# Two dense layers by Strassen's scheme: seven products of half blocks in place of eight, layer one ahead of layer two, squares held in DRAM

## The reference

```
h = x @ w_in          # 3072x512 by 512x2048
g = relu(h) ** 2
out = g @ w_out       # 3072x2048 by 2048x512
```

## Time and profile before

| what | value |
|---|---|
| median of three runs | 915.57 us |
| span of the profiled execution | 919.5 us |
| the profiled execution's own device time | not recorded beside its span |
| dense stage in it | 391.03 to 915.49 us |
| TensorE busy | 902.2 us, 98% |
| DVE, ACT busy | 473.0 and 423.6 us |
| DMA moved | 99.55 MB |

### The profile page before, as it was taken

How to read it: one execution, slowest core, us unless ns; L and a number is a source line. 1 busy time by engine, 2 the same in 40 slices (tenths; PEclk the granted TensorE clock), 3 DMA queues, 4 the chain that set the end, 5 groups by cost and what they waited for, 6 DMA issues and landing times.

```text
span 919.5 us, 17240 instructions
## 1 busy us (share of the span) xinstructions
PE 902.2 (98%) x5248; PEld 734.5 (80%) x5249; DVE 473.0 (51%) x1431; ACT 423.6 (46%) x978; POOL 92.2 (10%) x146
## 2 busy tenths in 40 slices
PE   9999999989899999999999999999999999999998
PEld 7878777767688887888888888888888888888886
DVE  5787899876566678763242224222422332243224
ACT  7888999855566668552232113211322221232123
POOL 3112222224222223100000000000000000000000
PEclk9999999999999999999999999999999999999999
DMA  5556775185677669740012003100400040004001
GB/s 200 172 166 201 234 230 172 69 302 199 222 251 248 224 220 357 260 96 0 1 52 41 1 0 75 17 0 0 91 0 0 0 91 0 0 0 91 0 0 46
DMA packets 87463, 99.55 MB, mean 108 GB/s; under 512 B 56189, under 2 KB 56317, under 8 KB 87408
## 3 DMA queue, kind: packets, MB, share of 16 engines
q1 hardware_dynamic: 81120, 83.07, 29.0%
q0 software_dynamic: 6000, 15.49, 4.9%
q10 hardware_dynamic: 288, 0.34, 0.1%
HBM read 77.72 MB, written 25.56 MB: 112 GB/s over the span
## 4 chain that ended last, share of the span: by engine, by line
PE 89%; issue 3%; DMA 3%; ACT 2%; DVE 2%; ACTq 1%; POOLq 1%; POOL 0%; DVEq 0%; SPq 0%
PE bank L1220 29%; PE bank L1193 28%; PE bank L1102 6%; PE bank L1083 6%; PE bank L930 4%; PE bank L985 4%; PE bank L958 4%; PE bank L996 1%; DMA routed<-pad_row 1%; PE bank L1091 1%; ACT prob L703 1%; PE bank L1010 1%; PE bank L978 1%; PE bank L1075 1%; DMA x_raw<-routed 1%
## 5 line engine op out<-in xcount | busy, mean ns | idle before, releaser
L1591 DVE TENSOR_TENSOR g<-relu_c 128x512 f32<-128x512 f32 x96 | 66.5, 693 | 340.1 <-ACT relu_c L873 340.1
L873 ACT ACTIVATE relu_c<-bank 128x512 f32<-128x512 f32 x96 | 57.5, 599 | 371.1 <-PE bank L1193 371.1
L1220 PE MATMUL bank<-w_hi,g_lo 128*128 128x512 f32 x384 | 150.1, 391 | 0.0
L1193 PE MATMUL bank<-x_hi,w_lo 128*128 128x512 f32 x384 | 149.6, 390 | 0.0
L1220 PE MATMUL bank<-w_hi,g_hi 128*128 128x512 f32 x384 | 149.4, 389 | 0.0
L1220 PE MATMUL bank<-w_lo,g_hi 128*128 128x512 f32 x384 | 149.4, 389 | 0.0
L1193 PE MATMUL bank<-x_hi,w_hi 128*128 128x512 f32 x384 | 149.4, 389 | 0.0
L1193 PE MATMUL bank<-x_lo,w_hi 128*128 128x512 f32 x384 | 146.5, 389 | 0.0
L703 ACT ACTIVATE prob<-score,neg_max 128x264 f32<-128x264 f32 (+1 forms) x192 | 94.0, 496 | 14.2 <-DVE neg_max L1283 14.1
L1546 DVE TENSOR_TENSOR w_lo<-w_raw,w_hi x70 | 82.0, 1221 | 10.5 <-ACT w_hi L816 7.1
L1220 PEld LDWEIGHTS bank<-w_hi,g_lo 128*128 128x128 f32 x384 | 72.1, 188 | 17.2 <-DVE g_lo L1598 2.5
(11 more groups left out here) (151 smaller groups left out, 1304.3 us busy)
## 6 DMA issues: line engine op xcount, KB each, us to landing
w_raw<-in_weights SPq DMA_DIRECT2D x80, 512.0 KB, 5.8
q_in<-in_qT SPq DMA_DIRECT2D x24, 256.0 KB, 3.3
v_in<-in_v SPq DMA_DIRECT2D x24, 256.0 KB, 3.6
x_rows<-x_row SPq DMA_DIRECT2D x24, 256.0 KB, 3.2
x_row<-x_rows SPq DMA_DIRECT2D x96, 64.0 KB, 2.5
k_in<-in_kT SPq DMA_DIRECT2D x23, 264.0 KB, 3.6
x_res<-routed POOLq DMA_DIRECT2D x15, 260.0 KB, 6.4
x_raw<-routed POOLq DMA_DIRECT2D x14, 260.0 KB, 6.2
```

The source lines that it names most:

```text
L873: eng.activation(relu_c[:, f % 2, :], hc_ps[f % 2][:, :], ACT.Relu).then_inc(s_crelu, 1)
L1193: return eng.matmul(hc_ps[f % 2][:, :], w[f // UNIT][:, f % UNIT, wcols], x[:, c, :], start=begins, stop=ends)
L1220: ins = eng.matmul(yc_ps[s][:, :], gg[:, f % 2, s * P:(s + 1) * P], w[f // UNIT][:, f % UNIT, DM:CH], start=(f == 0 and n == 0), stop=(f = ...
L1591: eng.tensor_tensor(g[:, f % 2, :], relu_c[:, f % 2, :], relu_c[:, f % 2, :], ALU.mult).then_inc(s_cg, 1)
```

## The change

`x` and `w_in` are cut into 2x2 blocks: token halves of 512, halves of the inner dimension of 256, column halves. With A the weights and B the tokens' blocks, sums of blocks are formed ahead, seven products are taken in place of eight, and the results are put together from them (Winograd's form). The same is done for the squares and `w_out`.

Layer one runs in 12 steps `t` (3 groups of 1024 tokens by 4 quarters of the hidden dimension). A step has seven products of 12 matmuls. Products 1 and 2 go to the banks `pa`, 5 and 3 to `pc`, 6 and 7 to `pb`, 4 to `pd`; the second one of a pair adds to what the first has left, after DVE or ACT has read it. Per step `p1_copy` (ACT) brings product 1 to `q1`; DVE makes `u2`, `u3_z22`, `z21`, `z12` in `q1` to `q3`; ACT makes ReLU and square of blocks 11, 22, 21 and 12 in place; and SP stores the four (128x1024 f32, 512 KB each) to `g_rows` in DRAM. `q1` and `q2` may be written again when their store has landed (`s_st21`, `s_st12`).

Layer two runs afterwards in 3 groups of 7 products of 4 units of 12 matmuls. SP loads the squares back (`chain_g`, `b12_g`, `stream_g`), DVE forms the block sums `t1` to `t4` and, per unit, the lower part (`unit_lower`); ACT makes the upper part (`unit_upper`), with a ring of three. Outputs are turned by DVE and stored in pieces of 128 bytes (`store_y`, four DMAs of 64 KB for each of 24 halves).

Of the weights, the first half of `w_in` is loaded during the last experts in place of the former units, and DVE makes its four sums (`first_sums`, ahead of the last expert). The other six slices pass through `w_in8`: SP loads one (`load_slice`, two DMAs of 512 KB), GpSimd makes four sums of 128x512 (`weight_sums`), ACT and DVE split seven blocks in three pieces (`slice_upper`, `slice_lower`) at t = 1, 2, 9, 10, 11 and after the last step. Slices for layer two overwrite those of layer one.

The core of the diff (block layout, buffers and layer two are left out):

```diff
+PRODUCTS = (1, 5, 6, 2, 7, 4, 3)
+LATER = {p: n + 1 for n, p in enumerate(PRODUCTS)}
+OPENING = (1, 2, 5, 6, 7, 4, 3)
+STEPS, QUARTERS, PIECES = 12, 4, ((1, 3), (3, 5), (5, 8))
...
+        PAIR = {"a": (0, 1), "c": (4, 5), "b": (6, 7), "d": (2, 3)}
+        pa, pc, pb, pd = (banks[:, n:m + 1, :] for n, m in PAIR.values())
+        BANK_OF = {1: "a", 2: "a", 5: "c", 3: "c", 6: "b", 7: "b", 4: "d"}
...
+            def store_g(t, blk, q, made, done):
+                eng.wait_ge(made, 2 * t + 2)
+                eng.dma_start(g_rows[t // QUARTERS, blk, t % QUARTERS, :, :], q[:, :, :].rearrange("p j t -> p (j t)")).then_inc(done, 16)
...
+            load_slice(0)
             eng.wait_ge(s_bscatter, tiles * 16 + 16)
             close(eng)
             eng.wait_ge(s_cturn, 4)
+            for c in range(DC):
+                load_x(0, 1, c, first_in[c], s_cx[c])
...
+            x_order = ((0, 0), (0, 1), (1, 0), (1, 1), (0, 2), (0, 3), (1, 2), (1, 3))
+            for t in range(STEPS):
+                if t in (2, 5):
+                    if t == 2:
+                        eng.wait_ge(s_wpl, 6)
+                    else:
+                        eng.wait_ge(s_xl, x_made(1, 3))
+                    for n, (token_half, c) in enumerate(x_order):
+                        load_x((t + 2) // 3, token_half, c, x_in[n], s_xin[n // 2])
+                if t == 9:
+                    eng.wait_ge(s_xl, x_made(2, 3))
+                    load_slice(2)
+                if t in (10, 11):
+                    load_slice(t - 7)
+                if t == STEPS - 1:
+                    for n in range(4):
+                        eng.wait_ge((s_st11, s_st12, s_st21, s_st22)[n], 16 * QUARTERS)
+                    load_chain(0, 0)
+                    load_chain(0, 1)
+                store_g(t, B11, q4, s_g11, s_st11)
+                if t == 1:
+                    eng.wait_ge(s_wpl, 3)
+                    load_slice(1)
+                if t in (9, 10):
+                    eng.wait_ge(s_wpl, 3 * (t - 6))
+                if t == STEPS - 1:
+                    load_chain(0, 2)
+                    load_chain(0, 3)
+                    eng.wait_ge(s_wpl, 15)
+                    load_slice(5)
+                store_g(t, B22, q3, s_g22, s_st22)
+                if t == STEPS - 1:
+                    load_b12(0, 0)
+                    load_b12(0, 1)
+                store_g(t, B21, q1, s_g21, s_st21)
+                if t == STEPS - 1:
+                    load_b12(0, 2)
+                    load_b12(0, 3)
+                store_g(t, B12, q2, s_g12, s_st12)
...
+            def weight_sums(k):
+                eng.wait_ge(s_win, 32 * k + 32)
+                a21, a11, s1, s2, a12, s3, a22, s4 = (w_in8[:, n, :] for n in range(8))
+                eng.tensor_tensor(s1, a21, a22, ALU.add).then_inc(s_wsum, 1)
+                eng.tensor_tensor(s3, a11, a21, ALU.subtract).then_inc(s_wsum, 1)
+                eng.wait_ge(s_wsum, 4 * k + 1)
+                eng.tensor_tensor(s2, s1, a11, ALU.subtract).then_inc(s_wsum, 1)
+                eng.wait_ge(s_wsum, 4 * k + 3)
+                eng.tensor_tensor(s4, a12, s2, ALU.subtract).then_inc(s_wsum, 1)
+            for k in range(6):
+                weight_sums(k)
...
+            def slice_upper(k, piece):
+                first, end = PIECES[piece]
+                s = (k + 2) % 4
+                if k >= 2:
+                    eng.wait_ge(s_one, halves(s + 8, 3 if k < 5 else (5, 2, 3)[piece]))
+                eng.wait_ge(s_wsum, 4 * k + 4)
+                eng.activation(w_hi[s // 2][:, first:end, s % 2 * SUPER:s % 2 * SUPER + SUPER], w_in8[:, first:end, :], ACT.Copy).then_inc(s_wph, 1)
+            def p1_copy(t):
+                eng.wait_ge(s_one, halves(t, 1))
+                wait(eng, s_st21, 16 * t)
+                eng.activation(q1[:, :, :], pa, ACT.Copy).then_inc(s_p1, 1)
...
+            eng.wait_ge(s_bscatter, tiles * 16 + 16)
+            close(eng)
+            for t in range(STEPS):
+                p1_copy(t)
+                if t == 0:
+                    block11(0)
+                    for p in (5, 6, 7, 4, 3):
+                        x_upper(0, p, x_source(0, p))
+                if t in (3, 7):
+                    x_upper((t + 1) // 4, 1, x_source(1, 1))
+                    x_upper((t + 1) // 4, 5, x_source(1, 5))
+                if t in (4, 8):
+                    x_upper(t // 4, 4, x_source(1, 4))
+                    x_upper(t // 4, 3, x_source(1, 3))
+                if t in (1, 2, 9, 10, 11):
+                    for piece in range(3):
+                        slice_upper({1: 0, 2: 1, 9: 2, 10: 3, 11: 4}[t], piece)
+                if t == STEPS - 1:
+                    unit_upper(0, 1, 0)
+                if t > 0:
+                    block11(t)
+                if t in (3, 7):
+                    x_upper((t + 1) // 4, 6, x_source(1, 6))
+                if t == STEPS - 1:
+                    unit_upper(0, 1, 1)
+                block22(t)
+                if t in (3, 7):
+                    x_upper((t + 1) // 4, 2, x_source(1, 2))
+                block21(t)
+                if t in (3, 7):
+                    x_upper((t + 1) // 4, 7, x_source(1, 7))
+                if t == STEPS - 1:
+                    unit_upper(0, 1, 2)
+                    slice_upper(5, 0)
+                block12(t)
+            slice_upper(5, 1)
+            slice_upper(5, 2)
...
+                if t >= 1:
+                    if p == 1:
+                        eng.wait_ge(s_g11, 2 * t - 1)
+                    elif p == 5:
+                        eng.wait_ge(s_z12, t)
+                    elif p == 6:
+                        eng.wait_ge(s_u3, 2 * t)
+                    elif p == 4:
+                        eng.wait_ge(s_z21, t)
+                if p == 2:
+                    eng.wait_ge(s_p1, t + 1)
+                elif p == 7:
+                    eng.wait_ge(s_u2, t + 1)
+                for j in range(2):
+                    if p == 3:
+                        eng.wait_ge(s_z22, 2 * t + j + 1)
+                    to = bank[PAIR[BANK_OF[p]][j]]
+                    for c in range(2):
+                        eng.matmul(to, w(w_lo, j, c), xh[p][:, c, :], start=(c == 0 and p in (1, 5, 6, 4)), stop=False, skip_group_check=True)
+                        eng.matmul(to, w(w_hi, j, c), xh[p][:, c, :], start=False, stop=False, skip_group_check=True)
+                    if s == 0 and j == 0:
+                        eng.wait_ge(s_xl, x_made(m, p))
+                    for c in range(2):
+                        ins = eng.matmul(to, w(w_hi, j, c), xl[p][:, c, :], start=False, stop=(c == 1), skip_group_check=True)
+                    ins.then_inc(s_one, 1)
...
+            def first_sums():
+                eng.wait_ge(s_landed, UNIT * (E - 2) + HEAD)
+                a21, a11, a12, a22, s1, s2, s3, s4 = (w_raw[:, n, :] for n in range(8))
+                eng.tensor_tensor(s3, a11, a21, ALU.subtract).then_inc(s_wsums, 1)
+                eng.tensor_tensor(s1, a21, a22, ALU.add).then_inc(s_wsums, 1)
+                eng.wait_ge(s_wsums, 2)
+                eng.tensor_tensor(s2, s1, a11, ALU.subtract).then_inc(s_wsums, 1)
+                eng.wait_ge(s_wsums, 3)
+                eng.tensor_tensor(s4, a12, s2, ALU.subtract).then_inc(s_wsums, 1)
...
+            def slice_lower(k, piece):
+                first, end = PIECES[piece]
+                s = (k + 2) % 4
+                eng.wait_ge(s_wph, 3 * k + piece + 1)
+                cols = slice(s % 2 * SUPER, s % 2 * SUPER + SUPER)
+                eng.tensor_tensor(w_lo[s // 2][:, first:end, cols], w_in8[:, first:end, :], w_hi[s // 2][:, first:end, cols].bitcast(F32), ALU.subtract).then_inc(s_wpl, 1)
...
+            def u2(t):
+                eng.wait_ge(s_one, halves(t, 6))
+                eng.wait_ge(s_p1, t + 1)
+                wait(eng, s_st12, 16 * t)
+                eng.tensor_tensor(q2[:, :, :], q1[:, :, :], pb, ALU.add).then_inc(s_u2, 1)
+            def u3_z22(t):
+                for j in range(2):
+                    eng.wait_ge(s_one, halves(t, 7, j))
+                    eng.tensor_tensor(q1[:, j, :], q1[:, j, :], bank[PAIR["b"][j]], ALU.add).then_inc(s_u3, 1)
+                for j in range(2):
+                    if j == 0:
+                        wait(eng, s_st22, 16 * t)
+                    eng.wait_ge(s_u3, 2 * t + j + 1)
+                    eng.tensor_tensor(q3[:, j, :], q1[:, j, :], bank[PAIR["c"][j]], ALU.add).then_inc(s_z22, 1)
+            def z21(t):
+                eng.wait_ge(s_one, halves(t, 4))
+                eng.wait_ge(s_z22, 2 * t + 2)
+                eng.tensor_tensor(q1[:, :, :], q1[:, :, :], pd, ALU.subtract).then_inc(s_z21, 1)
+            def z12(t):
+                eng.wait_ge(s_one, halves(t, 3))
+                eng.wait_ge(s_u2, t + 1)
+                eng.tensor_tensor(q2[:, :, :], q2[:, :, :], pc, ALU.add).then_inc(s_z12, 1)
...
+            x_lower(0, 1, pb)
```

(52 more changed lines are left out.)

568 lines of the change are left out of this document (386 added, 182 removed).

## The result

The changed kernel takes 923.31 us in the median of six runs (919.57 to 928.09), the kernel before 915.27 beside it: 1.009 times as long, 95% interval 1.0066 to 1.0114. So it is 8.0 us slower where 8.6 us less were forecast; 907 and the range to 920 are both missed, on the other side of no change.

The account below looks back on a forecast made before the run. TensorE, busy 98% of the span, was taken to bound the kernel. Terms -67.5 +3 +12.6 +10 +19.5 +9 +4.8 = -8.6 us took the median from 915.57 to 907 us; range 898 to 915, with rivals 889 to 920.

Parts of the forecast that it names:

- step 0: First step of layer one: second token half loaded late, product 5 waits; 31.6 us in place of 19.04, +12.6 (12 to 15.5).
- step 3: Layer one, t=3: block 21's store stands behind 32 loads, so `p1_copy` is late for product 2; +10 us (0 to 13).
- the end: After the last matmul: z12's pass, transposes, SP issues and landing, 8.8 us behind TensorE, now 4.0; +4.8 us.
- step 6: Layer one, t=6: the 32 loads from t=5 end 2.0 us into it, the copy is in time; 0 us.
- Rival 1: Store round trip decides: each of 11 steps waits on the stores of the step before; 919 us, chance 0.16.
- rival 4: DVE bounds layer two, at 1.45 us a pass; 916 us, no change, chance 0.06.
- Rivals 2 and 3: Rival 2 has its own line; the other: SP's issue costs nothing, so step 3 loses nothing; 897 us, chance 0.08.
- Steps 9 to 11: Late layer-one steps: weight slice's load and GpSimd sums delay z22, product 3 waits three times; +19.5 us (6 to 45).
- the clock: TensorE after a long idle wait: granted 0.50 of full speed, costing some 1.5 us more per wait.
- Rival 2: The weight preparation hides: GpSimd takes 0.8 us a sum, Steps 9 to 11 cost little; 885 to 892 us, chance 0.20.
- the transition: Between the layers: slice 5 loaded late, product 1's unit 3 begins at 14.1 and not 8.2 us; +9 (3 to 14).

Follow-up runs that it names:

- e2: The changed kernel with the 32 loads of `x` in steps 2 and 5 sent in groups between the four stores, not ahead of them: 923.15 us.
- e7: The changed kernel with three `t1` ahead of slice 5's lower parts and the fourth unit's upper part right behind the slice's first piece: 923.88 us.
- e11: The changed kernel with discarded multiplies in TensorE's waits, 30 ahead of the first step's product 5 and 26 ahead of the wait for slice 5: 921.96 us.
- e15: e13 with most of the last two pieces of slice 5's lower part left out, so its output is incomplete: 880.35 us.
- e12: Kernel of all changed orders with slice 5 early, summed by VectorE (886.76 us), plus sums ahead of the third unit's lower part and 14 discarded multiplies: 885.35 us.
- e13: e12 with the lower parts of product 5's first units placed between the `t1` sums on DVE: 888.42 us.

## Why the prediction was wrong

**The mechanisms.** The places named were there, each with the releaser named: the second half of `x` in step 0, `p1_copy` behind an SP store in step 3, three waits for z22 behind `slice_lower`, the fourth unit, the end. Only the wait in step 6 had not been named. So the mechanism was right and the sizes were not. Rival 1 did not come: a store lands 2.6 us after its issue in the median, and the groups of `u2` and `p1_copy` from 391 to 675 us (busy, mean ns, idle time before them) show 3.7 and 18.4 us of waiting for stores in all twelve steps, of which 3.7 and 17.2 in steps 3 and 6, behind the loads:

```profile
L1935 DVE TENSOR_TENSOR q<-q,banks 128x1024 f32<-128x1024 f32 x12 | 14.6, 1220 | 54.3 <-PE banks L1499 50.6 <-DMA g_rows<-q 3.7
...
L1086 ACT ACTIVATE q<-banks 128x1024 f32<-128x1024 f32 x12 | 12.2, 1020 | 20.9 <-DMA g_rows<-q 18.4 <-PE banks L1499 2.5
```

Nor did rival 4: in layer two beyond its first units, 12 matmuls take 2.72 us. Rivals 2 and 3 were wrong in the other direction. Slower came by a way that no rival had: the forecast's own waits, nearly all of them longer than priced.

**Steps 9 to 11, "it lands at 8.7, then GpSimd makes four 128x512 sums in a row": +25.6 in place of +19.5.** This step of the prediction failed most. The load landed 5.9 us after its issue, 10.3 us into the step; I had allowed 4.65, though the earlier trace rows gave 3.8, 6.0 and 10.3 for loads of that size. The sums took 5.2 us instead of 4.8, so that z22 came at 22.5 and not 20.9: 6.1 to 6.7 us of wait, not 5.0. And the clock took 1.7 to 2.2 us each time, not 1.5. The estimate from the Trainium skill's GPSIMD Engine Reference (section 3.1), 1.12 us, was further off than mine: 1.29 in the rows. Rival 2 rested on the bound from below, 0.8 us, and the sums took 1.6 times that. The step's own working has slips besides. From 16.3 to 20.9 it is 4.6 us, not 5.0; and with sums of 0.8 and 2.5 us put into the same chain its bounds come out near 10 and 35 us, not 6 and 45, so that rival 2, too, was priced too fast.

**Step 3, +13.8 in place of +10.** The 32 loads took 18.41 us, not 17.0 (one issue in their middle took 1.94 us), and the store behind them landed after 4.56 us where 2.8 was carried over from stores with nothing ahead. Together that is 3.2 of the 3.8 us. By e2 the reason given was half of it: DVE's transposes hold `u2` just as long, where the prediction let them delay it by 0.5.

**Step 6, +2.3 in place of 0.** "End at 2.0 us of step 6": they ended at 3.5, by the same 18.64 us, and the store landed after 4.53. The 1.5 us of slack that the prediction had worked out were less than these two errors.

**Step 0 and the transition, +1.9 and +2.8.** Product 5 began 15.7 us into the stage, 15.0 were forecast; most of the rest is the clock, which took 2.5 us where 1.5 were charged. This is no more than the spread of step 0 between executions (30.5 to 33.4 us), so nothing can be learned from its size. The slice landed 8.0 us after its issue at 670.59, while SP sent six more loads and three stores of 512 KB between 668.4 and 675.5, and the fourth unit began 16.9 us into layer two, 2.8 later than forecast. The second hold-up that the forecast had behind it, of product 5's first unit by three `t1`, did not show: 8.55 us of wait and 3.0 us of clock make nearly all of the 11.8. It was there beneath, as e7 and e11 to e15 showed: what bound next was DVE's sum of work.

**The clock** was charged 1.5 us a wait, from the one wait of 3.75 us in the earlier trace rows. Six waits of 6 to 11 us lost 1.7 to 3.0 us each by the windows, some 14 us in all; e11 gave back about half of step 0's, and nothing of the transition's.

**The range.** Four terms had bounds, and three came out inside them: step 0, steps 9 to 11 and the transition. Step 3, at 13.8, was just above its 13, and step 6 had been given none. Yet the time is outside the range, because that was cut at 920, well short of the sum of these bounds. The errors had causes partly in common, landings beside other traffic and the clock behind a wait, and six terms went the same way by 17.0 us, with 0.7 back at the end. The chance of 0.19 for slower was too small for that.

## What to carry to other kernels

A change that saves the bounding engine's work by adding stages to every other queue should be priced with the rows' median landing, not the shortest, and with one common error for all the terms that share a queue. Where two streams wait for the same late load, undoing one wait gives nothing (e2), and where one engine's row of work binds, another order only moves the wait (e7, e12, e13); follow each engine's order to the end before counting a return. The scheme itself was worth having: with slices sent a step ahead (e1) it is 2.2% faster than the kernel before (interval 1.9 to 2.5), and with the orders of e12, at 885.35 us, 3.1% (interval 2.9 to 3.3).
